# Recurrent attention with two expert layers: the old state added on VectorE, the first set scaled on VectorE, the last staging copies reordered

## The reference

```
for t in range(S):                       # S = 768, D = 40
    y[t] = r[t] @ state
    Sa = state @ a[t]
    state = state * w[t] - outer(Sa, b[t]) + outer(v[t], k[t])
x = y as [3072, 320]
x = moe(x)      # out = p(best) * sigmoid(x @ w_out)[best] * relu(x @ w1[best]) @ w2[best]
out = moe2(x)   # same without the sigmoid, at most `capacity` tokens per expert
```

## Time and profile before

| what | us |
|---|---|
| median of 3 runs | 1190.72 |
| the profiled execution | 1190.92 |
| its span on the engines | 1189.2 |
| PE busy | 1066.2 (90%) |
| PE weight load busy | 910.4 (77%) |
| DVE busy | 572.4 (48%) |
| ACT busy | 421.2 (35%) |
| POOL busy | 329.7 (28%) |
| granted TensorE clock, mean | 0.947 |
| opening, to the first product of the chain | 0 to 69.3 |
| rounds 0 to 11 of the chain | 69.3 to 503 |
| routing of layer 1, to its first tile | 505 to 531 |
| tiles of layer 1 | 531 to 831 |

### The profile page before, as it was taken

The page is one execution under the profiler, slowest core; times in us unless marked ns, Lnnn a source line. Parts: engine busy times, 40 slices in busy tenths (PEclk is TensorE's granted clock), DMA queues, the critical chain, the costliest instruction groups (busy, mean ns, idle before and its releaser), DMA issues.

```text
span 1189.2 us, 36969 instructions
## 1 busy us (share of the span) xinstructions
PE 1066.2 (90%) x16070; PEld 910.4 (77%) x16070; DVE 572.4 (48%) x864; ACT 421.2 (35%) x575; POOL 329.7 (28%) x279
## 2 busy tenths in 40 slices
PE   2489999899989899889999999997599999988997
PEld 1378888788878898758888888886378888866885
DVE  8555557856557552255677777768611111110111
ACT  0144444554444454314333333331033333323331
POOL 7343445434455310010222222222022222211220
PEclk7678899999999898989999999999799999988999
DMA  5244444454444432340333142331113133333000
GB/s 118 63 108 89 110 88 106 123 121 99 102 89 113 112 64 65 130 134 12 116 122 118 56 129 85 118 114 53 49 34 121 35 120 116 122 116 109 23 12 1
DMA packets 181906, 107.37 MB, mean 90 GB/s; under 512 B 136120, under 2 KB 164800, under 8 KB 181620
## 3 DMA queue, kind: packets, MB, share of 16 engines
q1 hardware_dynamic: 171600, 85.00, 27.5%
q0 software_dynamic: 6016, 16.05, 4.4%
q10 hardware_dynamic: 4132, 3.96, 1.0%
HBM read 87.51 MB, written 22.09 MB: 92 GB/s over the span
## 4 chain that ended last, share of the span: by engine, by line
PE 66%; SPq 16%; DMA 6%; DVE 4%; issue 4%; ACT 2%; POOL 1%; ACTq 0%; POOLq 0%; DVEq 0%
PE pair L1251 22%; PE pair L1232 19%; PE pair L1239 6%; SPq L423 5%; SPq L474 3%; SPq L455 3%; DMA t_dram<-T_rows 2%; PE pair L1219 2%; SPq L436 2%; PE pair L1101 2%; SPq L443 2%; PE bank L1114 2%; PE pair L1050 1%; SPq L483 1%; PE pair L1133 1%
## 5 line engine op out<-in xcount | busy, mean ns | idle before, releaser
L1251 PE MATMUL pair<-abk_own,H_nat 128*128 x992 | 277.8, 433 | 2.0 <-DVE S_nat L1537 1.7
L1232 PEld LDWEIGHTS pair<-H_nat,rvm 128*128 128x128 f32 x1984 | 237.5, 197 | 23.9 <-issue 12.5
L1232 PE MATMUL pair<-H_nat,rvm 128*128 128x128 f32 x1984 | 239.2, 281 | 12.7 <-issue 10.3
L1251 PEld LDWEIGHTS pair<-abk_own,H_nat 128*128 128x128 f32 x992 | 184.0, 190 | 71.8 <-issue 3.2
L722 ACT ACTIVATE rvm<-ring_own 128x2560 f32 x62 | 145.0, 2339 | 102.6 <-issue 80.4
L876 ACT ACTIVATE H_nat<-pair 128x512 f32<-128x512 f32 x62 | 37.0, 597 | 323.6 <-PE pair L1239 323.6
L1537 DVE TENSOR_SCALAR S_nat<-pair,gate_all 128x320 f32<-128x320 f32 x62 | 34.1, 551 | 206.2 <-PE pair L1251 206.2
L1530 DVE TENSOR_SCALAR H_nat<-pair 128x512 f32<-128x512 f32 x62 | 42.5, 686 | 167.3 <-PE pair L1239 152.0
L635 POOL TENSOR_SCALAR_AFFINE_SELECT AG<-AG 64x512 f32<-64x512 f32 x48 | 62.8, 1308 | 142.1 <-ACT AG L722 139.7
L703 POOL DMA_INDIRECT out<-S_nat,token_all x31 | 31.5, 1016 | 246.6 <-DVE S_nat L1537 238.6
L703 POOL DMA_INDIRECT between<-S_nat,token_all x31 | 33.9, 1094 | 233.8 <-DVE S_nat L1548 225.7
(11 more groups left out here) (142 smaller groups left out, 1448.2 us busy)
## 6 DMA issues: line engine op xcount, KB each, us to landing
abk_own<-w SPq DMA_DIRECT2D x16, 1280.0 KB, 8.7
ring_own<-w SPq DMA_DIRECT2D x16, 512.0 KB, 3.6
ring_own<-w SPq DMA_DIRECT2D x32, 256.0 KB, 4.5
t_dram<-T_rows SPq DMA_DIRECT2D x12, 384.0 KB, 3.6
ring_own<-w SPq DMA_DIRECT2D x32, 128.0 KB, 5.1
w_in<-wT SPq DMA_DIRECT2D x48, 80.0 KB
abk_own<-aT SPq DMA_DIRECT2D x24, 160.0 KB
abk_own<-bT SPq DMA_DIRECT2D x48, 80.0 KB
```

Of the source, the lines that this page charges most:

```text
L1232: mm(to, w1_now[:, par, k * F + m * P:k * F + m * P + P], xT[:, (0, 2 - m // 4)[k], :], start=(m % 4 == 0 and k == 0), stop=False, skip_gr ...
L1251: last = mm(bank[5][:, 0:DM], hidT[par][:, k, :], ring2[:, bass.ds(place, 1), k, :].rearrange("p a d -> p (a d)"), start=(k == 0), stop=(k ...
```

## The change

`state(u)` loses its two products with the identity; its 16 products write bank 7 alone. DVE's `state_out` first adds bank 7 and the old `Z_diag` into a new SBUF tile `Z_sum` (two instructions), waits for them, and makes `ZV` and `Z_diag` from `Z_sum` and the decay in place of bank 7 and the decay. All but two units have it: 22 of 24. The scaling of a, b and k of set 0 goes from POOL to DVE (`scale_set_0`, 4 + 2 instructions), behind the decays of set 0; the fills of `rvm` and `ZV` go from DVE to the end of POOL's fills. In ACT's `x_out` the logit parts are copied first, and in the last unit `x_out` goes ahead of `u_out`. The first routing has 9 fill products in place of 11.

```
-WARM = 11
+WARM = (9, 11)
...
+        Z_sum = sb("Z_sum", [P, 2 * NPAIR, D])
...
-            nc.gpsimd.memset(UV_even, 0.0).then_inc(cleared, 1)
+            for t in (UV_even, rvm[:, :], ZV[:, :]):
+                nc.gpsimd.memset(t, 0.0).then_inc(cleared, 1)
...
                 if grams:
-                    if gram_set == 0:
-                        scale_first(0)
...
-                    scale_a(2 * gram_set + 1)
+                    if gram_set:
+                        scale_a(2 * gram_set + 1)
...
+                    if u == NU - 1:
+                        x_out(j - 1)
                     if chain:
                         u_out(u)
                         ut_out(u)
-                    if c == 1 and 0 < j <= NK:
+                    if c == 1 and 0 < j <= NK and u != NU - 1:
                         x_out(j - 1)
...
-                pe.wait_ge(st_done, 2 * states_upto(u - 1))
-                pe.wait_ge(z_kept, 2 * states_upto(u - 1))
-                for o in range(2):
-                    mm(bank[7][head_rows(o), 0:H * D], ident[:, SIDE[o]:SIDE[o] + D],
-                       Z_diag[:, diag_of(u), :, SIDE[o]:SIDE[o] + D], start=True, stop=False, ...)
+                pe.wait_ge(st_added, 2 * states_upto(u - 1))
...
-                for t in (rvm, ZV):
-                    v.memset(t[:, :], 0.0).then_inc(cleared, 1)
...
+            def scale_set_0():
+                dve.wait_ge(f_scanned, 1)
+                dve.wait_ge(ag_cleared, 1)
+                dve.wait_ge(a_landed, 32)
+                for u in range(CC):
+                    for o in range(2):
+                        q = head_rows(o)
+                        v.tensor_tensor(AG[q, u, o]..., a_in[q, :, :, u * C:(u + 1) * C]...,
+                                        fruns(0)[q, u::CC, 0:C], ALU.mult).then_inc(a_scaled, 1)
+                dve.wait_ge(bk_landed[0], 128)
+                for u in range(CC):
+                    v.tensor_tensor(both, both, ends..., ALU.mult).then_inc(bk_scaled, 1)
...
                 dve.wait_ge(st_ready, states_upto(u))
+                dve.wait_ge(z_cleared, 1)
+                dve.wait_ge(z_kept, 2 * states_upto(u - 1))
+                for o in range(2):
+                    q = head_rows(o)
+                    v.tensor_tensor(Z_sum[q], view(7, 2 * NPAIR, D)[q],
+                                    Z_diag[q, diag_of(u), :, SIDE[o]:SIDE[o] + D], ALU.add).then_inc(st_added, 1)
                 dve.wait_ge(end_kept, k + 1)
+                dve.wait_ge(st_added, 2 * states_upto(u))
                 for o in range(2):
                     q = head_rows(o)
                     v.tensor_tensor(
-                        ZV[q, to % 4, o]..., view(7, 2 * NPAIR, D)[q],
+                        ZV[q, to % 4, o]..., Z_sum[q],
                         end_decay[q, k, c::CC]..., ALU.mult).then_inc(st_done, 1)
...
...
                 if j == SLOTS[0]:
+                    scale_set_0()
                     clear_rest()
```

More of the change, by code:

```diff
@@ L327, in recurrence_and_experts @@
         z_kept = sem("z_kept")
+        st_added = sem("st_added")
         z_cleared = sem("z_cleared")
@@ L662, in _ @@
                         pool.wait_ge(r_ready, 2 * gram_set - 3)
-                    scale_a(2 * gram_set + 1)
-                    pool.wait_ge(bk_landed[gram_set % 2], 128 * (gram_set // 2 + 1))
-                    for u in (2 * gram_set, 2 * gram_set + 1):
-                        scale_bk(u)
+                    if gram_set:
+                        scale_a(2 * gram_set + 1)
+                        pool.wait_ge(bk_landed[gram_set % 2], 128 * (gram_set // 2 + 1))
+                        for u in (2 * gram_set, 2 * gram_set + 1):
+                            scale_bk(u)
                 if nats:
@@ L797, in x_out @@
                     act.wait_ge(x_written[k % 2], 32 * (k // 2))
[L798 to L801, removed]
                 if k >= 2:
@@ L805, in x_out @@
                      pair[2][:, :, :].rearrange("p b (a t) -> p b a t", t=P)[:, :, :, D:D + 2 * E], x_copied)
+                for b in range(2):
+                    copy(x_stage[:, k % 2, b, :].rearrange("p (a o d) -> p a o d", a=NPAIR, o=2),
+                         pair[2][:, b, :].rearrange("p (a o d) -> p a o d", a=NPAIR, o=2)[:, :, :, 0:D], x_copied)
             def write_x(k):
@@ L1073, in state @@
             def state(u):
-                pe.wait_ge(st_done, 2 * states_upto(u - 1))
-                pe.wait_ge(z_kept, 2 * states_upto(u - 1))
-                for o in range(2):
-                    mm(bank[7][head_rows(o), 0:H * D], ident[:, SIDE[o]:SIDE[o] + D],
-                       Z_diag[:, diag_of(u), :, SIDE[o]:SIDE[o] + D], start=True, stop=False, skip_group_check=True)
+                pe.wait_ge(st_added, 2 * states_upto(u - 1))
                 pe.wait_ge(u_copied, 2 * (u + 1))
@@ L1084, in state @@
                             last = mm(bank[7][head_rows(o), at:at + D], H_nat[:, u % 4, o, b, a, :],
-                                      ZV[:, u % 4, o, b, a, :], start=False, stop=True, skip_group_check=True)
+                                      ZV[:, u % 4, o, b, a, :], start=True, stop=True)
                 last.then_inc(st_ready, 1)
@@ L1202, in _ @@
                 last.then_inc(L["count_ready"][s], 1)
-                fill(WARM)
+                fill(WARM[s])
                 for g in range(NG):
@@ L1307, in decays @@
                                      0.0, ALU.mult, ALU.add).then_inc(f_scanned, 1)
+            def scale_set_0():
[5 more added lines that the diff above has]
+                        q = head_rows(o)
+                        v.tensor_tensor(
+                            AG[q, u, o].rearrange("p b a t -> p (b a) t"),
+                            a_in[q, :, :, u * C:(u + 1) * C].rearrange("p b a t -> p (b a) t"),
+                            fruns(0)[q, u::CC, 0:C], ALU.mult).then_inc(a_scaled, 1)
+                dve.wait_ge(bk_landed[0], 128)
+                for u in range(CC):
+                    both = bk_in[0].rearrange("p b a c r t -> p (b a) c r t")[:, :, u]
+                    ends = E_run[:, 0, 2:].rearrange("p (n t) -> p n t", t=C + 1)[:, u::CC, 0:C]
+                    v.tensor_tensor(both, both, ends.unsqueeze(2).to_broadcast([P, 2 * NPAIR, 2, C]), ALU.mult
+                                    ).then_inc(bk_scaled, 1)
             def solve_first(k):
@@ L1369, in state_out @@
                     v.tensor_tensor(
-                        ZV[q, to % 4, o].rearrange("p b a d -> p (b a) d"), view(7, 2 * NPAIR, D)[q],
+                        ZV[q, to % 4, o].rearrange("p b a d -> p (b a) d"), Z_sum[q],
                         end_decay[q, k, c::CC].unsqueeze(2).to_broadcast([D, 2 * NPAIR, D]), ALU.mult
                         ).then_inc(st_done, 1)
-                dve.wait_ge(z_cleared, 1)
                 for o in range(2):
@@ L1376, in state_out @@
                     v.tensor_tensor(
-                        Z_diag[q, diag_of(to), :, SIDE[o]:SIDE[o] + D], view(7, 2 * NPAIR, D)[q],
+                        Z_diag[q, diag_of(to), :, SIDE[o]:SIDE[o] + D], Z_sum[q],
                         end_decay[q, k, c::CC].unsqueeze(2).to_broadcast([D, 2 * NPAIR, D]), ALU.mult
```

## The result

The changed kernel takes 1236.78 us (median, 1232.97 to 1239.44) against 1191.13 for the one before; the ratio is 1.0389 with a 95% interval of 1.0327 to 1.0451. That is 45.7 us slower, where 25.4 were forecast. The profiled execution took 1232.97 us, with a span of 1231.2. A median in this text holds every execution, while a ratio leaves out those few that ran in a slower state of the chip, so where the two differ the ratio counts.

The account below looks back on a forecast made before the run. PE was taken to bound the attention. State +31.5, less 3.2 for the opening, 1.1 for ACT's order and 1.8 for the fill, gave +25.4 us on 1190.9, that is 1216; range 1186 to 1238, the forecast's own 1206 to 1228.

Parts of the forecast that it names:

- the shared port: In ten even units, DVE products with two SBUF inputs stand still until POOL's reading instruction ends; 33.2 us.
- 31.5: State part in total: 33.2 us in even units plus 7.7 us at corners, less 9.4 us of covered waits.
- the rival with the clock: PE stands still longer and its clock falls: six more falls at some 3 us, 1234 us; chance 0.09.
- the term of 33.2 us: Ten even units where POOL scales: its instructions go in between DVE's products and delay right_side, 1.8 to 4.6 us each.
- DVE holds its place: In even units DVE keeps its place for all four products against POOL; about 17 us, total 1205; chance 0.16.
- The corner: Odd units: DVE's additions delay the mask that the corner waits for; nine corners x 0.85, 7.7 us.
- 7.7 - 9.4: Corner delay of 7.7 us, less PE's waits for POOL's b, k (5.1) and T (4.3), taken as covered.
- I take zero: Removing state(u)'s two identity products from PE wins nothing, since ACT's copy of u covers them; 0 us.
- a gain of 16: Rival that the two removed products were on the path: PE has 16 us less to do, 1169; chance 0.10.
- The opening: Set 0 scaled on DVE while POOL fills: gram matrix sent at 25.7, gain 3.2 us, between 2.2 and 4.6.
- ACT's order: Last unit: the three copies that inner waits for go ahead of u_out; gain 1.1 us, at most 1.4.
- The fill: First routing: fewer fill products let sorting start and end 1.8 us earlier; gain 1.8, or 0.

Follow-up runs that it names:

- the sum in PSUM: Changed kernel, but DVE's sum is made in place in PSUM bank 7 instead of SBUF; 1208.68 us, ratio 1.0201 to the kernel before.
- the ladder: Three kernels on the kernel before, one chip: DVE's additions in bank 7 with two unread PE products; without those; sum in SBUF. Ratios 1.0027, 1.0121, 1.0340.
- The additions alone: Kernel before, with DVE adding the old state in bank 7 and PE keeping two products that nothing reads; 1195.98 us, ratio 1.0027.
- the hole-only run: Kernel before without its two identity products on PE, DVE's instructions unchanged, old state left out of the result; 1202.18 us, ratio 1.0052.
- the ladder's second profile: Kernel before, with DVE adding the old state in bank 7 and no identity or unread products on PE; 1206.36 us, ratio 1.0121.
- its third: Kernel before with the whole state part of the change, the sum in SBUF, and no other part; 1232.14 us, ratio 1.0340.
- the state part alone: Kernel before with only the state part: identity products gone, DVE adds into SBUF, products from SBUF; 1236.24 us, ratio 1.0434; on another chip 1.0340.
- with the fills guarded: Kernel before with set 0 scaled on DVE, ACT's new order, and GpSimd's moved fills waiting for DVE's first decay copy; 1187.13 us, ratio 0.9962.
- the run of the opening: Kernel before with set 0 scaled on DVE, rvm and ZV filled by GpSimd, ACT's new order, 11 fill products; 1183.70 us, ratio 1.0009.

## Why the prediction came out as it did

The direction and the place were right, and so was the mechanism that was forecast, the shared port. But it is only a part of what happened. In the profile PE's waits cost 11 us where 31.5 were added up for them, and the larger part of the loss, 33 us of a lower clock, stood in the sum at nothing (both are worked out below). That the measured 1236.8 lies in the range of 1186 to 1238 is in part luck, for it lies outside the forecast's own 1206 to 1228 and nearest to the rival with the clock (1234, chance 0.09). The forecast was too small by 20 us.

**Products with two SBUF inputs.** Right, and shown: the sum in PSUM takes the wait away and by the ratios 22 us with it (1.0389 and 1.0201, on two chips), and the ladder, on one chip, gives 25.8. Unit 0 went as walked through: 3.32 us for the forecast 3.45, with POOL between the two rows of heads. But the term of 33.2 us was mis-sized. Of the ten even units, POOL's second b, k instruction went in between the two products in only four (units 0, 6, 12 and 14, with waits of 3.32, 3.26, 3.16 and 3.27 us). In these the first product was issued beside POOL's first instruction, and "DVE holds its place" has fallen with them. In the other six the products came when the second instruction was already running, a mask at most went in between, and they cost `right_side` 4.3 us together. So it waited 17.3 us (21.0 in the ladder) against some 22. The other 11 us of the term, behind `right_side`, came to nothing in the changed kernel's list and to 0.3 us in the ladder: POOL's masks take only about 0.3 us from each of DVE's `Z_diag` products in unit 0, and `right_side` itself was longer at the lower clock. What made up for it is the clock.

**The corner.** The wait grew by 5.9 us, from 2.1 to 8.0, for the forecast 7.7. The additions alone, with the waits for POOL and T that they cover, cost 2.8 us in the ladder (at most 6.4 by the interval), where the prediction's 7.7 - 9.4 gives a gain of 1.7. Waits don't add up one by one: the step took each as paid or won in full.

**The step that failed: "I take zero".** The two products were costed at nothing because ACT's copy covers them. The cover is there, and the hole costs 10.4 us in the ladder and 6 in the hole-only run, through the clock. A bound from both sides was written for it, zero and a gain of 16; a loss wasn't in it. The trace of before shows no round without these products, but it does show that in a round with a fall of the clock PE is busy for 2.3 us longer (35.86 against 33.58, of the 3.9 us that the round takes more).

**The clock as a rival.** It stood beside the forecast with a chance of 0.09, as if it were another way. It comes on top of the hole and of the waits at `right_side`; with the corners' waits alone the clock stayed at 0.96. At the lower of the two levels, 1.2 GHz, the chain spent about 35 us before and about 114 after (what the mean clock lacks, 0.04 and 0.12, times two and the chain's 433 and 477 us). PE's busy time says what that cost: 397.1 less the 17.0 us of the removed products is 380.1, and it was 413.0, so 33 us of the chain's 44 are the same products at a lower clock. The other 11 are the idle time that grew, 28.1, less the 17.0 that the products no longer fill. The port's part is mixed as well: from the ladder's second profile to its third PE's idle time grew by 20.6 us (51.8 to 72.4) and its busy time, with the same products, by 12.7. That split is rough, since the second profile is of the fastest of six executions. Why the clock falls at holes of about 1 us is not shown by any run.

**The opening.** Right in the profile: the first `right_side` moved from 69.3 to 66.1, 3.2 us, and the gram matrix was sent at 26.02 for the forecast 25.7. Not foreseen was that the copy of the decays can stand behind the moved fills; it is a copy in SBUF, and the prediction looked only at scans beside fills.

**ACT's order.** Right: from the start of `solved` to `inner` 4.41 us before and 3.36 after, 1.05 won.

**The fill.** Forecast a gain of 1.8; the changed kernel lost: sorting began earlier in the routing by 1.6 us, and then took 2.9 longer at the lower clock. On its own the part is within the noise. It isn't so each time: of the six profiles with nine fills two show the sorting at the lower clock (8.38 us) and four near 5.5, while all eight with eleven fills show 5.46 or 5.47. What decides it with nine stays open.

The three small parts together were taken as 6.1 us of gain. The changed kernel (1.0389) and the state part alone (1.0434 and 1.0340 on two chips) are not far enough apart to show any of it. That too stays open for the changed kernel; on the kernel before, with the fills guarded, it is 0.4%.

The rule of the Trainium skill that the prediction weighed ("SBUF — State Buffer", "Who interferes with whom") is borne out by the products' 1108 ns against 489. That a GpSimd instruction which only writes leaves DVE's two-input products alone, as it says, holds as well: the four products that scale a took 2.84 us beside the fill of `rvm`, and 2.84 in the run of the opening, from 20.47, where no fill was left. The other rule weighed there ("VectorE: DVE Perf Modes", "Two Vector instructions with no wait between them") fits unit 0 too: the second product, on rows that start in another quadrant (a group of 32 partitions), left POOL its turn.

## What to carry to other kernels

Before moving arithmetic to DVE, ask where both inputs of each product will lie: here an input left in PSUM kept DVE free of GpSimd, and the same sum in SBUF cost 26 us. A product on TensorE that fills a wait is not always free to remove: here what was gone as work came back as clock. Where DVE copies within SBUF, don't queue long GpSimd fills in front of it without a wait.

## What the runs showed of the hardware that was not expected

A DVE copy in SBUF of 128x16 elements, which took 0.11 us in each of the eleven later sets of the changed kernel, stood for 7.68 us behind GpSimd fills that only write, through two more fills back to back (to 20.42), in one execution; in another for 5.42, through one more; in others it got in after the one that was running, in 1.18 to 1.38. It ended 0.03 us after a fill each time: at 20.42, 18.25 and, in the changed kernel, 13.94, with fills that end at 20.39, 18.22 and 13.91. It was the same code, so whether DVE gets in between two fills that follow without a wait isn't fixed. That it is the shared port that held the copy was argued, not shown on its own; the wait that keeps the fills behind the copy does take the delay away (1.24 us).

With the two products gone and nothing else changed, the longest wait at their place went from 0.4 to 1.1 us, the clock in the chain went from 0.96 to 0.90, and PE took 10 us more of busy time for 17 us less of products.
